# Two groups of spare products in the first attention, the second batch's key exponentials behind two K+ tiles, and other copies of numerators and output rows

## The reference

```python
def phi(x):
    proj = np.einsum('bhsd,df->bhsf', x, w_phi)
    proj = proj - np.max(np.abs(proj), axis=-1, keepdims=True)
    return np.concatenate([np.exp(proj), np.exp(-proj)], axis=-1)
q_p, k_p = phi(q), phi(k)
kv, z = einsum('bhsf,bhsd->bhfd', k_p, v), sum(k_p, axis=2)
x = einsum('bhsf,bhfd->bhsd', q_p, kv) / (einsum('bhsf,bhf->bhs', q_p, z)[..., None] + 1e-06)
...
xk = mu_k * x + (1.0 - mu_k) * x_prev      # and xr with mu_r; x_prev is x one token earlier
k = np.maximum(xk @ w_k, 0.0)
y = sigmoid(xr @ w_r) * (k * k @ w_v)
...
h = np.maximum(y @ w_in, 0.0)
out = (h * sigmoid(conv3(h)) @ w_out)
```

## Time and profile before

| | us |
|---|---|
| median of 3 runs | 1289.95 (1288.88 to 1289.97) |
| profiled execution, its own time | 1286.36 |
| its span, first to last instruction | 1284.6 |
| PE busy | 1265.4 |
| DVE busy | 816.4 |
| ACT busy | 563.1 |
| POOL busy | 142.8 |

### The profile page before, as it was taken

How to read it: one execution, slowest core, us unless ns; L and a number is a source line. 1 busy time by engine, 2 the same in 40 slices (tenths; PEclk the granted TensorE clock), 3 DMA queues, 4 the chain that set the end, 5 groups by cost and what they waited for, 6 DMA issues and landing times.

```text
span 1284.6 us, 23638 instructions
## 1 busy us (share of the span) xinstructions
PE 1265.4 (99%) x9506; PEld 1081.3 (84%) x9506; DVE 816.4 (64%) x1334; ACT 563.1 (44%) x1072; POOL 142.8 (11%) x137
## 2 busy tenths in 40 slices
PE   8889999999999999999999999999999999999998
PEld 6668887888788879788878878999899898898996
DVE  6788576576566766667657666546484583672852
ACT  4653634525434354353443544454344353352441
POOL 2512111102111211121111211000000000000000
PEclk8999999999999999999999999999999999999999
DMA  5512211221222222222131220422102102012001
GB/s 163 163 40 74 65 49 47 83 68 31 79 59 60 61 57 59 69 59 59 41 88 39 60 78 12 134 70 68 70 1 79 48 23 78 1 70 79 1 34 41
DMA packets 91540, 79.03 MB, mean 62 GB/s; under 512 B 61864, under 2 KB 70184, under 8 KB 90408
## 3 DMA queue, kind: packets, MB, share of 16 engines
q1 hardware_dynamic: 91272, 77.46, 19.9%
q10 hardware_dynamic: 160, 0.07, 0.0%
HBM read 58.21 MB, written 19.01 MB: 60 GB/s over the span
## 4 chain that ended last, share of the span: by engine, by line
PE 90%; DVE 3%; issue 3%; DMA 2%; ACT 1%; SPq 0%; ACTq 0%; DVEq 0%
PE psm L574 36%; PE ps L574 22%; PE psh L1197 6%; PE psh L1198 6%; PE psh L1196 6%; PE pso L1198 5%; PE pso L1196 5%; PE pso L1197 5%; PE ps L686 1%; DMA den<-den_scr 1%; ACT k_signs L826 1%; DMA den_scr<-den_cols 1%; DVE q_part L969 0%; DMA phi<-in_w_phi 0%; DVE mix L1034 0%
## 5 line engine op out<-in xcount | busy, mean ns | idle before, releaser
L574 PE MATMUL psm<-xy_hi,wk_hi 128*128 128x288 f32 x512 | 156.4, 306 | 6.6 <-DVE xy_lo L1053 3.9
L574 PE MATMUL psm<-k_hi,wv_hi 128*128 128x288 f32 x512 | 153.8, 300 | 0.0
L1198 PE MATMUL psh<-xy_hi,win_lo 128*128 128x288 f32 x512 | 151.3, 296 | 0.0
L1196 PE MATMUL psh<-xy_hi,win_hi 128*128 128x288 f32 x512 | 151.3, 296 | 0.0
L1197 PE MATMUL psh<-xy_lo,win_hi 128*128 128x288 f32 x512 | 151.3, 296 | 0.0
L574 PE MATMUL psm<-xy_lo,wk_hi 128*128 128x288 f32 x512 | 151.1, 295 | 0.0
L574 PE MATMUL psm<-k_lo,wv_hi 128*128 128x288 f32 x512 | 150.9, 295 | 0.0
L574 PE MATMUL psm<-k_hi,wv_lo 128*128 128x288 f32 x512 | 150.8, 295 | 0.0
L574 PE MATMUL psm<-xy_hi,wk_lo 128*128 128x288 f32 x512 | 150.7, 294 | 0.0
L1320 DVE SCALAR_TENSOR_TENSOR conv<-h,taps,conv 128x576 f32<-128x576 f32 x64 | 52.1, 814 | 138.8 <-ACT conv L1275 138.8
L562 POOL TENSOR_TENSOR z_pairs<-k_signs 128x512 f32<-128x512 f32 x56 | 73.2, 1307 | 601.7 <-ACT k_signs L826 597.7
(11 more groups left out here) (147 smaller groups left out, 2830.2 us busy)
## 6 DMA issues: line engine op xcount, KB each, us to landing
k_in<-in_k SPq DMA_DIRECT2D x32, 320.0 KB, 3.3
v_nat<-in_v SPq DMA_DIRECT2D x32, 320.0 KB, 3.6
q_in<-in_q SPq DMA_DIRECT2D x32, 288.0 KB, 3.1
y_scr<-y SPq DMA_DIRECT2D x64, 144.0 KB, 2.5
y<-y_scr SPq DMA_DIRECT2D x8, 1152.0 KB, 5.8
den<-den_scr SPq DMA_DIRECT2D x60, 144.0 KB, 3.0
out<-rows SPq DMA_DIRECT2D x32, 256.0 KB, 2.0
stage<-in_moe_w_in SPq DMA_DIRECT2D x4, 512.0 KB, 4.0
```

The lines of the kernel that those rows point to most:

```text
L574: return nc.tensor.matmul(o, lhsT, rhs, start=first, stop=last, skip_group_check=True)
L1196: nc.tensor.matmul(o, wh, xh, start=first, stop=False, skip_group_check=True)
L1198: return nc.tensor.matmul(o, wl, xh, start=False, stop=last, skip_group_check=True)
```

## The change

It has six edits.

- The 7 spare products at the start become 8, and two groups of 4 are put into the first attention of pair 0: one between the queries of pair 1 and KV0, one between KV1 and PICK.
- In the list of batch 0's iteration, EK and EL of batch 1's pair 0 leave their place ahead of the K tiles and stand behind the tiles K+ 0 and K+ 1.
- The numerator of pair 1 of the first batch is copied into `square` and not into `num`, and no longer waits until DVE has divided pair 0.
- For pairs 2 and 3 of the first batch ACT copies the first half of the denominator, the numerator, and the second half of the denominator, as three instructions instead of two; DVE's halves wait for their own half.
- In phase 2, DVE copies the token tiles 1 and 3, ACT the tiles 0, 2 and 4, and `rows_ready` becomes `even_rows` and `odd_rows`.
- In the last round, tile 4 is made in two halves of 256 columns in two banks, each copied and stored by itself.

```diff
-WARM_FIRST, WARM = 7, 6
+WARM_FIRST, WARM = 8, 4
...
-    steps = [("G", 0), ("F", 0), ("EK", 0), ("F", 1), ("QT", 0), ("KV0", 0), ("M", 0)] + hi()
-    steps += [("EL", 0)] + hi() + [("QT", 1), ("KV1", 0), ("PICK", 0)] + hi() + lo() + lo()
+    steps = [("G", 0), ("F", 0), ("EK", 0), ("F", 1), ("QT", 0), ("WARM", 0), ("KV0", 0), ("M", 0)] + hi()
+    steps += [("EL", 0)] + hi() + [("QT", 1), ("KV1", 0), ("WARM", 0), ("PICK", 0)] + hi() + lo() + lo()
...
 BESIDE_SECOND = {
     **BESIDE_NEXT,
+    ("K+", 0, 0): [("EK", 0)],
+    ("K+", 0, 1): [("EL", 0)],
...
-            else:
+            elif step not in (("EK", 0), ("EL", 0)) or batch:
                 emit(step)
...
+    def numerator(p, a):
+
+        return square[:].rearrange("p i s -> p (i s)") if (p, a) == (1, 0) else num[:]
...
         def copy_wide(p, a):
             await_(act, attended, PAIRS, a, p + 1)
+            nc.scalar.activation(den_first[:, p - WIDE, 0:HALF], q_cols(1, p, a)[:, 0:HALF], ACT.Copy, bias=1e-6).then_inc(first_den, 1)
             nc.scalar.activation(num_first[:, p - WIDE, :], q_cols(0, p, a), ACT.Copy).then_inc(num_copied, 1)
-            nc.scalar.activation(den_first[:, p - WIDE, :], q_cols(1, p, a), ACT.Copy, bias=1e-6).then_inc(first_den, 1)
+            nc.scalar.activation(den_first[:, p - WIDE, HALF:S], q_cols(1, p, a)[:, HALF:S], ACT.Copy, bias=1e-6).then_inc(first_den, 1)
...
         def copy_num(p, a):
             await_(act, attended, PAIRS, a, p + 1)
-            await_x(act, p, a)
-            nc.scalar.activation(num[:], q_cols(0, p, a), ACT.Copy).then_inc(num_copied, 1)
+            if (p, a) != (1, 0):
+                await_x(act, p, a)
+            nc.scalar.activation(numerator(p, a), q_cols(0, p, a), ACT.Copy).then_inc(num_copied, 1)
...
-            dve.wait_ge(first_den, own + 1)
+            dve.wait_ge(first_den, 2 * own + n + 1)
...
+    def last_columns(c):
+
+        halves = slice(0, DM // 2), slice(DM // 2, DM)
+        return halves if c == TWOS - 1 else (slice(0, DM),)
...
-    def o_bank(t):
-
-        return pso[:, t, :] if t < 4 else psh[:, 1, 1, :]
+    def o_bank(t, n=0):
+
+        return pso[:, t, :] if t < 4 else psh[:, 1, 1 - n, :]
...
-                for j in range(FT):
-                    last = out_part(0, 4, j)
-                last.then_inc(out_done, 1)
+                for n, cols in enumerate(last_columns(c)):
+                    for j in range(FT):
+                        last = out_part(0, 4, j, cols, n)
+                    last.then_inc(out_done, 1)
...
-            nc.scalar.activation(rows[:, t, :], o_bank(t), ACT.Copy, scale=0.5).then_inc(rows_ready, 1)
+            for n, cols in enumerate(last_columns(c) if t == 4 else (slice(0, DM),)):
+                act.wait_ge(out_done, token_tiles(c, half, t + 1 + n))
+                nc.scalar.activation(rows[:, t, cols], o_bank(t, n)[:, cols], ACT.Copy, scale=0.5).then_inc(even_rows, 1)
...
-            for t in range(4 + half):
+            for t in range(0, 4 + half, 2):
                 copy_rows(c, half, t)
...
+        def copy_rows(c, half, t):
+            dve.wait_ge(out_done, token_tiles(c, half, t + 1))
+
+            if c > 0:
+                dve.wait_ge(stored[t], c * 32 + 16 * half)
+            elif half:
+                dve.wait_ge(stored[t], 16)
+            nc.vector.tensor_scalar(rows[:, t, :], o_bank(t), 0.5, None, ALU.mult).then_inc(odd_rows, 1)
...
+            for t in (1, 3):
+                copy_rows(c, half, t)
```

More of the change, by code:

```diff
@@ L410, in await_bank @@
             if u:
-                eng.wait_ge(first_den, PAIRS - WIDE)
+                eng.wait_ge(first_den, 2 * (PAIRS - WIDE) + u - 2)
             return
@@ L999, in divide @@
             await_(dve, r_mixed, 2 * XT, a, 0)
-            nc.vector.tensor_tensor(x[:, p, 1:1 + S], num[:], den[:], ALU.mult).then_inc(x_ready, 1)
+            nc.vector.tensor_tensor(x[:, p, 1:1 + S], numerator(p, a), den[:], ALU.mult).then_inc(x_ready, 1)
         def divide_half(n, p):
             cols, own = slice(HALF * n, HALF * n + HALF), p - WIDE
-            dve.wait_ge(first_den, own + 1)
+            dve.wait_ge(first_den, 2 * own + n + 1)
             nc.vector.reciprocal(den_first[:, own, cols], den_first[:, own, cols]).then_inc(first_inverse, 1)
@@ L1139, in phase_2 @@
         sem("gated_ready"), sem("g_hi_ready"), sem("g_lo_ready"))
-    out_done, rows_ready = sem("out_done"), sem("rows_ready")
+    out_done, even_rows, odd_rows = sem("out_done"), sem("even_rows"), sem("odd_rows")
     stored = [sem(f"stored{t}") for t in range(TT)]
@@ L1152, in token_tiles, with await_rows, await_all_rows @@
         return c * TILES + (4 * half + n)
+    def await_rows(eng, c, half, t):
+        eng.wait_ge((even_rows, odd_rows)[t % 2], c * (4 + (t + 1) % 2) + 2 * half + t // 2 + 1)
+    def await_all_rows(eng, c, half):
+        eng.wait_ge(even_rows, 5 * c + 2 * half)
+        eng.wait_ge(odd_rows, 4 * c + 2 * half)
+    def last_columns(c):
+        halves = slice(0, DM // 2), slice(DM // 2, DM)
+        return halves if c == TWOS - 1 else (slice(0, DM),)
     def y_tiles(c, half, n):
@@ L1170, in store @@
             for t in range(4):
-                sp.wait_ge(rows_ready, token_tiles(c, half, t + 1))
+                await_rows(sp, c, half, t)
                 sp.dma_start(out[c * 2 + half][P * t:P * t + P, :], rows[:, t, :]).then_inc(stored[t], 16)
             if half:
-                sp.wait_ge(rows_ready, token_tiles(c, 1, 5))
-                sp.dma_start(out[c * 2 + 1][4 * P:S, :], rows[0:TAIL, 4, :]).then_inc(stored[4], 16)
-                sp.dma_start(out[c * 2][4 * P:S, :], rows[TAIL:P, 4, :]).then_inc(stored[4], 16)
+                for n, cols in enumerate(last_columns(c)):
+                    await_rows(sp, c, 1, 4 + 2 * n)
+                    sp.dma_start(out[c * 2 + 1][4 * P:S, cols], rows[0:TAIL, 4, cols]).then_inc(stored[4], 16)
+                    sp.dma_start(out[c * 2][4 * P:S, cols], rows[TAIL:P, 4, cols]).then_inc(stored[4], 16)
         def load_y(b):
@@ L1188, in sync @@
         store(TWOS - 1, 1)
-        for s in stored:
+        for s in stored[0:4]:
             sp.wait_ge(s, 16 * B)
+        sp.wait_ge(stored[4], 16 * B + 32)
     def tensor(pe):
@@ L1198, in three, with out_part @@
             return nc.tensor.matmul(o, wl, xh, start=False, stop=last, skip_group_check=True)
-        def out_part(at, t, j):
+        def out_part(at, t, j, cols=slice(0, DM), n=0):
             tok = slice(at + P * t, at + P * t + P)
-            return three(o_bank(t), (g_hi[:, j, tok], g_lo[:, j, tok]), (wout_hi[:, j, :], wout_lo[:, j, :]), j == 0, j == FT - 1)
+            return three(o_bank(t, n)[:, cols], (g_hi[:, j, tok], g_lo[:, j, tok]), (wout_hi[:, j, cols], wout_lo[:, j, cols]), j == 0, j == FT - 1)
         def batch(c, half):
@@ L1208, in batch @@
                 elif j == 1 and not half and c > 0:
-                    pe.wait_ge(rows_ready, token_tiles(c, 0, 0))
+                    await_all_rows(pe, c, 0)
                 cols = slice(P * j, P * j + P)
@@ L1221, in batch @@
             else:
-                pe.wait_ge(rows_ready, token_tiles(c, half, 0))
+                await_all_rows(pe, c, half)
             for j in range(FT):
```

2 lines of the change are left out of this document (1 added, 1 removed).

## The result

The changed kernel takes 1279.86 us (median of 5 runs, 1279.27 to 1282.27), the kernel before 1289.97 us (5 runs, 1288.88 to 1292.05): 0.9923 of it, 95% interval 0.9908 to 0.9937. The profiled execution took 1280.67 us and has a span of 1278.9 us against 1284.6 us: the profiles differ by 5.7 us, the medians by 10.1.

A forecast was written before the change was run, and what follows sets the result against it. PE was taken as the bound, busy 1265.4 of 1284.6 us. Terms summed to -4.0 us, taken as -4.4 with a few tenths for DVE meeting POOL less: 1289.95 to 1285.5 us, range for 8 in 10 1282.4 to 1288.5.

The forecast's parts named there:

- Idle time alone does not explain it: First attention: PE's idle time alone was said not to explain the granted clock's fall to 0.50 at 18 to 20 us.
- There the gap stands among wide products, here among narrow ones: Reason given why the clock held at 44 to 48 us but fell at 18 to 20 us; no size.
- The 3.6 us between the profile and the median: Median of the kernel before above its profiled execution; unexplained, carried over to forecast the changed kernel's median.
- The numerator in `square`: Pair 1's numerator copied without waiting for DVE's division, so PE's wait ahead of pair 3's queries goes: -1.3 us.
- The two groups: Spare products around KV0 and KV1 of pair 0 keep the clock up: -1.8 us, ends 0 and -2.7.
- The eighth product: Extra spare product at the start, filling most of a 0.6 us gap before the first keys: taken as 0.
- the early rise: Rival: without the start's gap the clock rises sooner; 1.4 us more gain, 1284.1 us, chance 0.10.
- The denominator in two pieces: Two ACT copies: EL of pair 3 later, +0.2 us; DVE's reciprocal for pair 3 starts at once, -0.2 us.
- The chain of f = 3: DVE's chain before the first K+ product, freed from POOL's z_pairs: -2.0 us, ends 0 and -2.5.
- The signs on ACT: EK and EL delay ACT's relu, so PE waits at the third whole K tile: +1.0 us.
- DVE beside POOL: Shared ports: k_lo up to 1.3 us late each, covered; small copies missing POOL's subtractions gain a few tenths.
- The end: Tile 4 in halves: products +0.3 us, smaller last copy -0.2, together +0.1 us; up to 0.2 less for the store.

The follow-up runs named there:

- e7: Kernel before with only the two exponentials EK and EL moved behind the K+ tiles: 1287.03 us, ratio 0.9976.
- e1: Kernel before, unchanged, run again to list each execution's mean clock: 1289.78 us, ratio 1.0011.
- e4: Kernel before with all spare products only (eight at the start and both groups of four): 1288.75 us, ratio 0.9996.
- e10: Changed kernel with pair 1's numerator in `num` again, so that its copy waits as before: 1285.32 us, ratio 0.9981.
- e13: Kernel before with all spare products and eight more ahead of pair 3's queries, the wait for the numerator kept: 1285.63 us, ratio 0.9969.
- e15: Changed kernel with pair 1's numerator in `num` again and eight spare products in the wait ahead of pair 3's queries: 1283.07 us, ratio 0.9949.
- e9: Changed kernel, unchanged, run again to list each execution's mean clock: 1279.56 us, ratio 0.9939 against the kernel before.
- e6: Kernel before with only pair 1's numerator copied into `square`: 1284.73 us, ratio 0.9968.
- e3: Kernel before with only the two groups of four spare products, seven still at the start: 1289.43 us, ratio 1.0009.
- e5: Changed kernel without the two groups and with seven spare products at the start: 1281.23 us, ratio 0.9938 against the kernel before.
- e14: Changed kernel without the two groups of four, the eighth product at the start kept: 1281.04 us, ratio 0.9928 against the kernel before.
- e11: Changed kernel with the exponentials EK and EL ahead of the K tiles again: 1281.81 us, ratio 0.9953 against the kernel before.
- e2: Kernel before with only the eighth spare product at the start: 1287.07 us, ratio 0.9992.
- e12: Changed kernel with DVE's division of pair 0 behind pair 3's maxima and pair 1's reciprocal: 1279.47 us, against 1279.56 us for the changed kernel beside it.
- e8: Kernel before with only the phase 2 edits (DVE's row copies, tile 4 in halves): 1290.33 us, ratio 1.0015.

## Why the prediction was wrong

The direction and most places were right; the size was off by 5.7 us, and it lies in two steps, both about the clock. Against the profiled execution alone the forecast was short by 1.3 us only, 1.07 of it the start.

- **The step that failed:** "Idle time alone does not explain it, for between 44 and 48 us PE was busy only 2.68 of 4.00 us, with a gap of 1.26 us ahead of pair 3's queries, at a clock of 1.00". One execution's clock was taken as what this gap always does. In six of eight profiles in which this gap is open it is followed by 0.50, in e7 at 0.95 us, in e1, e4 and e10 at 2.1 to 2.5 us. Filling it without touching the wait gives 3.1 us in e13 and 2.3 us in e15 (3.5 and 4.1 us by the ratios): shown. The reason given, "There the gap stands among wide products, here among narrow ones", fails with it: the gap of 2.7 to 2.8 us ahead of the first K+ product lies among products of 288 columns, and the clock falls there in five of nine profiles.
- **The 3.6 us between the profile and the median** were carried over as if they belonged to both kernels ("No row explains these 3.6 us"). They belong to the kernel before: 66 of its 103 executions have a mean clock of 0.993 or less and take 1289.5 us, 17 have 0.996 and take 1285.3 us. The changed kernel has 0.998 or more in all 13 executions of the result and of e9. The remark that a longer low clock would let the change gain more was right and was given no price.
- **"The numerator in `square`", -1.3 us,** was mis-sized. The wait ends with DMA and DVE and does not move with PE as a whole: in e1 PE starts KV0 of pair 2 at 38.94 us, 3.21 us sooner than in before, but pair 3's queries only 2.17 us sooner, and the wait is 2.32 instead of 1.26 us; in e10 it is 2.50 us. Alone the edit gave 4.1 us (e6), in the changed kernel 5.4 to 5.8 (e10), of which 1.3 to 3.5 are not the clock (e15).
- **The two groups, -1.8 us:** as summed in the profile, 2.89 - 1.07 us. They keep the clock up at the first gap, as forecast, in all eight profiles that have them and a fast start. But without the other edits they gave nothing by the medians beside them (e3), or with the eighth product 0.5 us (e4, -2.3 to +1.3); in e4's profile the clock falls at 44 us instead, behind the next gap. In the changed kernel they are worth 0 to 2 us, not separated from the noise (e5, e14).
- **The eighth product, 0:** wrong in the profile, where the early rise, a rival with 0.10, gave 1.07 us: the first pair's queries ran at the full clock. The ten profiles with eight products all have it, and so have three of the six with seven; so the product probably mends a slow start that some executions have and others not. Two executions with eight, 1288.79 us in e11 and 1291.13 us in e15, are 8 us above the others at a mean clock of 1.000, so it may not do so always. What it is worth in the median, e2 could not tell.
- **The denominator in two pieces, +0.2 and -0.2:** KV1 of pair 3 waited 0.29 us against 0.23, and the reciprocal no longer waits. Not tried by itself.
- **The chain of f = 3, -2.0 with the -0.2 before:** -2.2 us in the profile (6.01 - 3.78), with mix at 0.52 and xy_hi at 0.31 us as forecast. Taking the edit back costs 2.3 us (e11); of the stretch from the first K product to KV, 11.56, 12.79 and 14.13 us, 1.2 us are the edit and, in that profile, 1.3 the fallen clock.
- **The signs on ACT, +1.0 us:** 1.0 us in sum, but as 0.26 and 0.18 us of wait at two tiles and slower starts, not one wait of 1 us.
- **DVE beside POOL:** k_lo paid 0.3 us at most (0.75 us at 77.84 us, against 0.46 us). DVE's division at 42.93 us paid 2 us, where the prediction had only "a few tenths"; it ended 0.6 us after POOL's subtraction. The rule of the Trainium skill (SBUF — State Buffer, section Who interferes with whom), by which the loser waits for the whole instruction, agrees with that row.
- **The end, +0.1 us:** -0.5 us. The 256-column products come every 0.1185 us (1269.52 to 1275.09 by 47), and the last copy starts 5.88 us after the first product instead of 5.81, so PE pays under 0.1 us where 0.3 were taken; the copy takes 0.38 instead of 0.60 us, and what follows it 3.1 instead of 3.4 us. The estimate of 107 ns from the Trainium skill (TensorE: Matmul & The Clock Gate, section LDWEIGHTS), by which a load of 128 columns does not bound these products, agrees with that spacing. KV's 0.127 us a record was misread: 2.28 us by 18 counts the tail of the last record too, while from KV1 at 16.12 us to the group behind it at 18.14 us a record takes 0.112 us.

So the 10.1 us are 3.6 us by which the profile of before was a lucky one, 5.7 us between the profiles (1.1 start, 1.8 groups, 1.4 numerator (4.33 - 2.89), less 0.5 at DVE's meeting with POOL, 2.2 chain, less 1.0 signs, 0.5 end, and 0.2 in between), and 0.8 us by which the changed kernel's profile is above its median.

No version tried was faster than the changed kernel; e12 is the same.

## What to carry to other kernels

Where a kernel's executions differ by more than the sum you are working out, list the mean clock of each before pricing a wait: one profile shows one of several courses. A gap of PE of 1 to 3 us costs its own length and, in some executions and not in others, a stretch at half the clock behind it; so price all such gaps together, and expect that an edit that closes the first of them may bring nothing until the next is closed. Where PE waits for something that does not move with it, part of a gain upstream goes into that wait.

## What the runs showed of the hardware that was not expected

- The granted clock in the records can read 1.00 where PE runs slowly from the start: in e8 and e3 the queries took 3.14 and 3.15 us at a recorded 1.00, against 1.79 us. Five executions of before had a mean clock above 0.996 and yet took 1290.2 us. The Trainium skill (TensorE: Matmul & The Clock Gate, the caveats in the section Seeing it yourself) calls the trace events of the clock unreliable; these rows agree, and the durations decide.
- Eight spare products of 128x128, 1.95 us long, in a gap of 2.7 to 2.8 us kept the clock up in 11 of 12 executions of e13 (0.997 or more) and in all 12 of e15 (0.998 or more). Pair 3's queries started at 43.22 us with them (e15) and at 43.05 us without (e10).
- Gaps as short as 0.95 us (e7) were followed by half the clock, and one of 2.83 us (e8) was not.
- DVE behind a POOL subtraction of 2.4 us lost up to 2 us, and moving the DVE operation moved the meeting to the next one (e12).
